# Seven products instead of eight blocks of matmuls for six of twelve pairs of the second MoE's first matrix

## The chip, the cores and the metric

The kernel runs on one core of a Trainium2 chip. The metric is the device time of one execution in microseconds (us). Before the change it is 970.91, the median of three runs (968.33 to 972.44).

## The reference, cut to what matters

Attention with decay gives x, 3072 tokens of 512 features. A gated MoE layer (512 to 1536 to 512) follows, and then the layer with which this case deals:

```python
def _moe2_ref(x, w_in, w_out, g_ln):      # x: 3072 x 512, w_in: 512 x 1024, w_out: 1024 x 512
    h = x @ w_in
    e = np.exp(h - np.max(h, axis=-1, keepdims=True))
    solu = h * (e / (np.sum(e, axis=-1, keepdims=True) + 1e-09))
    mu = np.mean(solu, axis=-1, keepdims=True)
    var = np.mean((solu - mu) ** 2, axis=-1, keepdims=True)
    ln = (solu - mu) / np.sqrt(var + 1e-06) * g_ln
    return (ln @ w_out).astype(np.float32)
```

## The kernel before

All matrices are float32, and each factor is split into a high part (fp32r, made by ScalarE) and a low part (the rest, made by VectorE); a product is three matmuls: high x high, high x low, low x high. The first stage (attention and the gate and value matrices) and the second (the MoE's down matrix) compute 2 x 2 blocks of matrices by seven products of sums (Strassen's method as Winograd ordered it) in place of eight. The second stage writes its result to `x_dram`, by GpSimd's queue (`store_x2`), while ScalarE and VectorE convert operands into a ring of seven units, ahead of TensorE.

The last stage starts at 700 us. It works on 24 blocks of 128 tokens, named (tile, block): six tiles of four. For a block there is an **up** (`both_up`: two halves of 512 features, four contractions, three matmuls each, 24 matmuls of 128x512, into a PSUM bank each) and a **down** (`both_down2`, 24 matmuls of 128x512). Between them: ScalarE copies h out of PSUM (`copy_h`, L1284), VectorE takes the row maximum (L1724), ScalarE the exponent with its sum (L1288), VectorE the softmax product (L1738) and the mean, ScalarE the sum of squares (`square_solu`, L1317) and for two blocks together the square root (`deviation_of_pair`, with an activation table load before it and before the next exponent), VectorE normalises (L1760) and transposes within 32x32 blocks into z (L1770). When all four blocks of a tile are in z, sixteen DMAs on the sync engine's queue (`move_turned`, L690) move z into `ln_t`, four for each block to come. Then ScalarE makes `ln_t_hi` (L1298), VectorE `ln_t_lo` (L1775), and TensorE does the down; ScalarE copies the result (`scale_out`, L1343) into one of two buffers, from which SP stores it (L647). Tile 0 differs: TensorE transposes its blocks by itself (L1029).

The order is written out by hand for every engine. Ups run six blocks ahead of downs. Tile 0's step does the ups of the blocks up to (2,1). From tile 1 on, step (t,j) does the up of the block `run_up_of(t, j)`, six further on, and the down of (t,j); the other engines have per step one list each in `stage_c`. The last ups, of (5,2) and (5,3), stand in the steps (4,0) and (4,1); from (4,2) on only downs are left (`tail` on ScalarE). SP's queue holds, for each tile: two loads of `x_raw` (`load_pair`, 256 tokens each), the stores of finished blocks, and the sixteen moves of the next tile; for tile 5 the moves are in two halves around the store of (4,2). z has two buffers (`z_of`), one for even and one for odd tiles; `x_raw`, `x_hi` and `x_lo` have two buffers each.

## Time and profile before

| | |
|---|---|
| median of three runs | 970.91 us |
| profiled execution | 976.88 us, its span 975.1 |
| PE busy in the span | 944.7 us (97%), 5334 matmuls |
| VectorE, ScalarE, GpSimd busy | 644.2, 521.7, 136.4 us |
| mean granted TensorE clock | 0.989 of full speed |
| last stage | from 700 to 975 us |

PE is TensorE's matmuls, PEld its weight loads, DVE VectorE, ACT ScalarE, POOL GpSimd, SP the sync engine; SPq stands for what SP's queue issues. A timeline gives the start in us from the span's start, the duration, and in brackets how long the engine was idle and for whom. Matmuls overlap in the records: their spacing is their cost.

### The profile page before, as it was taken

What the parts mean: (1) busy time and instruction counts of PE and PEld (TensorE: products, weight loads), DVE (VectorE), ACT (ScalarE), POOL (GpSimd) and SP (SyncE); (2) the same over time, 40 slices, a digit from 0 to 9 for tenths busy, and PEclk for the clock granted to TensorE, in tenths of its full rate; (3) what the DMA queues carried; (4) which work ended last, traced back from release to release, by engine and by line L of the source; (5) the groups of instructions that cost most, each with busy time, mean ns of one, the idle gap of its engine ahead of it and who ended that gap; (6) DMA issues with size and microseconds to landing.
All of it is one profiled execution on the core that took longest, in us unless ns stands there. A gap on an engine that the chain in (4) does not pass through costs nothing.

```text
span 975.1 us, 14652 instructions
## 1 busy us (share of the span) xinstructions
PE 944.7 (97%) x5334; PEld 834.8 (86%) x5334; DVE 644.2 (66%) x1065; ACT 521.7 (54%) x911; POOL 136.4 (14%) x170
## 2 busy tenths in 40 slices
PE   8979999999999999999999999999999999999996
PEld 4666787787899999999999999999888888888875
DVE  3677895786778754454679877777375766666651
ACT  3554644554556433342546554555477866666641
POOL 4313301101115430000053101010100000000000
PEclk9799999999999999999999999999999999999998
DMA  9656545626153423131364616340510054351533
GB/s 271 194 168 201 171 165 164 194 114 189 48 215 115 157 80 121 50 127 52 131 226 146 235 57 232 111 166 25 179 57 32 20 143 91 94 128 46 110 85 86
DMA packets 103847, 126.61 MB, mean 130 GB/s; under 512 B 8160, under 2 KB 84320, under 8 KB 103776
## 3 DMA queue, kind: packets, MB, share of 16 engines
q1 hardware_dynamic: 98320, 109.28, 36.5%
q0 software_dynamic: 4736, 15.73, 4.7%
q8 instruction: 43, 0.70, 0.3%
q10 hardware_dynamic: 720, 0.66, 0.2%
q14 instruction: 28, 0.23, 0.1%
HBM read 77.41 MB, written 37.75 MB: 118 GB/s over the span
## 4 chain that ended last, share of the span: by engine, by line
PE 81%; DVE 7%; DMA 3%; issue 3%; ACT 2%; SPq 2%; POOL 0%; DVEq 0%; ACTq 0%; POOLq 0%
PE psum L949 11%; PE psum L952 11%; PE psum L951 11%; PE psum L385 7%; PE psum L386 7%; PE psum L387 7%; PE psum L985 6%; PE psum L987 6%; PE psum L988 6%; PE psum L842 3%; PE psum L876 3%; PE psum L866 2%; PE psum L855 2%; SPq L690 1%; DMA out<-out_buf 1%
## 5 line engine op out<-in xcount | busy, mean ns | idle before, releaser
L949 PE MATMUL psum<-xo_hi,w_hi 128*128 128x384 f32 x560 | 194.8, 348 | 6.5 <-DVE psum L1658 2.5
L951 PE MATMUL psum<-xo_lo,w_hi 128*128 128x384 f32 x560 | 187.9, 336 | 0.0
L952 PE MATMUL psum<-xo_hi,w_lo 128*128 128x384 f32 x560 | 187.9, 336 | 0.0
L949 PEld LDWEIGHTS psum<-xo_hi,w_hi 128*128 128x128 f32 x560 | 105.7, 189 | 12.7 <-DVE c L1662 4.4
L951 PEld LDWEIGHTS psum<-xo_lo,w_hi 128*128 128x128 f32 x560 | 105.7, 189 | 0.8 <-issue 0.3
L952 PEld LDWEIGHTS psum<-xo_hi,w_lo 128*128 128x128 f32 x560 | 105.4, 188 | 0.0
L1163 ACT ACTIVATE xo_hi<-b 128x768 fp32r<-128x768 f32 x84 | 70.7, 846 | 63.2 <-PE psum L988 52.4
L1538 DVE TENSOR_TENSOR xo_lo<-b,xo_hi 128x768 fp32r<-128x768 f32 x84 | 81.3, 970 | 34.6 <-ACT xo_hi L1163 34.4
L385 PE MATMUL psum<-w_in_hi,x_hi 128*128 128x512 f32 x192 | 75.9, 395 | 2.0 <-ACT h_buf L1284 2.0
L1658 DVE TENSOR_TENSOR psum<-psum,p_buf 128x384 f32<-128x384 f32 x48 | 27.1, 565 | 76.0 <-PE psum L952 76.0
L385 PE MATMUL psum<-w_out_hi,ln_t_hi 128*128 128x512 f32 x192 | 75.1, 391 | 1.2 <-DVE ln_t_lo L1775 1.2
L386 PE MATMUL psum<-w_in_lo,x_hi 128*128 128x512 f32 x192 | 75.5, 393 | 0.0
L387 PE MATMUL psum<-w_in_hi,x_lo 128*128 128x512 f32 x192 | 75.3, 392 | 0.0
L985 PE MATMUL psum<-xo_hi,w_hi 128*128 128x384 f32 x224 | 74.8, 334 | 0.0
L987 PE MATMUL psum<-xo_lo,w_hi 128*128 128x384 f32 x224 | 74.8, 334 | 0.0
L988 PE MATMUL psum<-xo_hi,w_lo 128*128 128x384 f32 x224 | 74.8, 334 | 0.0
L386 PE MATMUL psum<-w_out_lo,ln_t_hi 128*128 128x512 f32 x192 | 74.8, 389 | 0.0
L387 PE MATMUL psum<-w_out_hi,ln_t_lo 128*128 128x512 f32 x192 | 74.7, 389 | 0.0
L1484 DVE TENSOR_TENSOR probs<-psum,mask_t 128x256 f32<-128x256 f32 x96 | 40.5, 423 | 45.4 <-PE psum L842 44.3
L1123 ACT ACTIVATE x_tile<-psum 128x128 f32<-128x128 f32 x96 | 26.4, 275 | 76.7 <-PE psum L876 65.5
L842 PE MATMUL psum<-kq_buf 128*128 128x256 f32 x192 | 60.9, 400 | 0.8 <-DMA kq_buf<-q_t 0.7
L1190 ACT ACTIVATE silu<-psum 128x384 f32<-128x384 f32 x48 | 23.5, 491 | 65.1 <-PE psum L952 64.5
(142 smaller groups left out, 2030.2 us busy)
## 6 DMA issues: line engine op xcount, KB each, us to landing
act_dram<-act_buf SPq DMA_DIRECT2D x48, 384.0 KB, 2.4
b<-act_dram SPq DMA_DIRECT2D x48, 384.0 KB, 4.8
ln_t<-z SPq DMA_DIRECT2D x80, 128.0 KB, 3.1
kq_buf<-k_t SPq DMA_DIRECT2D x32, 192.0 KB, 2.7
kq_buf<-q_t SPq DMA_DIRECT2D x64, 96.0 KB, 3.0
q_dec<-q_t SPq DMA_DIRECT2D x32, 192.0 KB, 2.5
w_raw<-weights POOLq DMA_DIRECT2D x12, 512.0 KB, 5.1
x_dram<-x_tile SPq DMA_DIRECT2D x4, 1536.0 KB, 6.0
```

Source lines behind the costliest of these rows:

```text
L385: pe.matmul(dst, w_hi, m_hi, start=start, stop=False)
L386: pe.matmul(dst, w_hi, m_lo, start=False, stop=False)
L387: return pe.matmul(dst, w_lo, m_hi, start=False, stop=stop)
L842: pe.matmul(psum[:, SCORES[ch % 2], 0:2 * P], kq_buf[:, s, i, 0:P], kq_buf[:, s, i, P:3 * P], start=True, stop=True).then_inc(scores_done, 1)
L949: pe.matmul(dst, hi[:, cols], xo_hi[:, i, kc, :], start=i in (P1, P7) and kc == 0, stop=False, skip_group_check=True)
L951: pe.matmul(dst, hi[:, cols], xo_lo[:, i, kc, :], start=False, stop=False, skip_group_check=True)
L952: mm = pe.matmul(dst, lo[:, cols], xo_hi[:, i, kc, :], start=False, stop=kc == HK - 1, skip_group_check=True)
L985: pe.matmul(dst, hi[:, cols], xo_hi[:, u, c % 2, :], start=i in (P1, P7) and c == 0, stop=False, skip_group_check=True)
L987: pe.matmul(dst, hi[:, cols], xo_lo[:, u, c % 2, :], start=False, stop=False, skip_group_check=True)
L988: mm = pe.matmul(dst, lo[:, cols], xo_hi[:, u, c % 2, :], start=False, stop=c == FC // 2 - 1, skip_group_check=True)
L1163: act.activation(xo_hi[:, u % PRODUCTS, :, :], operand(u), ACT.Copy).then_inc(d_hi_ready, 1)
L1538: dve.tensor_tensor(xo_lo[:, u % PRODUCTS, :, :], operand(u), xo_hi[:, u % PRODUCTS, :, :].bitcast(F32), ALU.subtract).then_inc(d_lo_ready, 1)
```

## The change

Blocks 12 to 23 (tiles 3, 4 and 5), six pairs, get their up by seven products of a pair: the 256 tokens and 512 contractions are a 2 x 2 of blocks on the one side, contractions and the 1024 output features on the other. A product is two contractions of three matmuls of 128x512. The pair k takes P1, P7, P6, P2, P5 in an even step and P3, P4 in the odd step behind it, in the steps where its two ups stood. The last pair (k = 5) runs all seven in its first step, (4,0), in the order P1, P7, P6, P2, P5, P4, P3, and the lists of ScalarE and VectorE for (4,0) and (4,1) are written anew.

The sums of the weights (T) are made once by GpSimd in the second stage (eight pieces of 128x512, each stored to DRAM, later loaded again and converted by ScalarE and VectorE, two at a time, in tile 0 and the steps (1,0) and (1,1)). The sums of x (S) are made by GpSimd for each pair (`make_s`, four adds of 256 columns), its conversions are 512 + 256 + 1024 columns in three parts (`s_high`, `s_low`) in place of one of 1024. Between products ScalarE copies P1 within PSUM (`copy_xy`) and P7 out of it (`copy_p7`), VectorE adds twice (`add_u3`, `add_c22`); the four quarters of h reach `h_buf` by three copies and the second sum. There is one raw buffer for x in these pairs, loaded (`load_up`) when the whole operand of the pair before is converted, and only one z: the first transposition of a tile waits until all moves of the tile before have landed. The buffers of z1, the second x2 set and `d_squares` give the room. Sums, loads and conversions not shown below follow the same form.

```diff
+        UP_ORDER = (P1, P7, P6, P2, P5, P3, P4)
+        FIRST_PAIR = 6
+        PAIRS = C_TILES * BLOCKS // 2 - FIRST_PAIR
+        S_OF = {P1: 0, P2: 1, P4: 2, P5: 3, P6: 4, P7: 5, P3: 6}
+        T_PIECES = [(p, a) for p in (P7, P6, P5, P4) for a in range(HK)]
...
+        def pair_up(t, j):
+
+            k = (t * BLOCKS + j - BLOCKS) // 2 + 5 - FIRST_PAIR
+            return k if 0 <= k < PAIRS else None
...
+        def up_done(k, i):
+            order = UP_ORDER if k < PAIRS - 1 else UP_ORDER[0:5] + (P4, P3)
+            return PRODUCTS * k + order.index(i) + 1
...
                         sp.wait_ge(x2_stored[s], DMA * 2)
+                    sp.wait_ge(t_summed, len(T_PIECES))
...
-            def load_pair(t):
-
-                for g in range(2):
-                    sp.wait_ge(x2_lo_ready, 2 * (t - 1) + g + 1)
-                    load_x2(g, t)
+            def load_up(k):
+
+                if k > 0:
+                    sp.wait_ge(s_lo_ready, 3 * k)
+                else:
+                    sp.wait_ge(x2_lo_ready, 5)
+                load_x2(0, 2, k)

             def stage_c(t):
                 if t == 0:
...
-                if t + 2 < C_TILES:
-                    load_pair(t + 2)
-                store_out(t - 1, 3)
                 for j in range(3):
+                    if j % 2 == 0 and pair_up(t, j) is not None and pair_up(t, j) + 1 < PAIRS:
+                        load_up(pair_up(t, j) + 1)
+                    if j == 0:
+                        store_out(t - 1, 3)
                     if (t, j) == (C_TILES - 2, 2):
                         move_turned(t + 1, (0, 1))
...
+                pool.tensor_tensor(t_sum[:], first, second, ALU.subtract).then_inc(t_summed, 1)
+                pool.wait_ge(t_summed, at + 1)
+                pool.dma_start(t_store(T_PIECES.index((p, a))), t_sum[:]).then_inc(t_stored, DMA)
+
+            T_SUMS = [(p, a) for a in range(HK) for p in (P5, P6, P4, P7)]
+
...
+            def make_s(k):
+
+                raw = x2_raw[0]
...
+                if k > 0:
+                    pool.wait_ge(s_lo_ready, 3 * k)
+                    pool.wait_ge(s_made, 4 * k)
+                pool.tensor_tensor(s1, a21, a22, ALU.add).then_inc(s_made, 1)
+                pool.wait_ge(s_made, 4 * k + 1)
+                pool.tensor_tensor(s2, s1, a11, ALU.subtract).then_inc(s_made, 1)
...
+            for i in range(4):
+                load_t(i)
+            make_s(0)
+            for i in range(4, len(T_PIECES)):
+                load_t(i)
+            for k in range(1, PAIRS):
+                make_s(k)


...
+            def up_product(k, i):
+
+                if i in (P1, P2):
+                    pe.wait_ge(s_lo_ready, 3 * k + 1)
+                else:
+                    pe.wait_ge(s_lo_ready, 3 * k + 3)
+                if k == 0 and i in (P4, P5, P6, P7):
+                    pe.wait_ge(t_lo_ready, T_PIECES.index((i, HK - 1)) + 1)
+                if i == P1:
+                    at_least(pe, up_c11_copied, k)
+                elif i == P7:
+                    at_least(pe, up_c21_copied, k)
+                elif i in (P6, P2):
+                    pe.wait_ge(up_xy_copied, k + 1)
+                elif i in (P5, P4):
+                    pe.wait_ge(up_u3_ready, k + 1)
+                else:
+                    pe.wait_ge(up_c22_ready, k + 1)
+                dst = psum[:, {P1: UX, P2: UX, P7: UV, P4: UV}.get(i, UY), :]
+                for a in range(HK):
+                    x_hi, x_lo = s_hi[:, S_OF[i] * HK + a, :], s_lo[:, S_OF[i] * HK + a, :]
+                    m_hi, m_lo = up_weight(i, a)
+                    pe.matmul(dst, x_hi, m_hi, start=i in (P1, P7) and a == 0, stop=False, skip_group_check=True)
+                    pe.matmul(dst, x_hi, m_lo, start=False, stop=False, skip_group_check=True)
+                    mm = pe.matmul(dst, x_lo, m_hi, start=False, stop=a == HK - 1, skip_group_check=True)
+                mm.then_inc(up_product_done, 1)
+
...
-                        both_up(*run_up_of(t, j))
+                    if (t, j) in ((1, 0), (1, 1)):
+                        both_up(2, j + 2)
+                    if pair_up(t, j) is not None:
+                        whole = pair_up(t, j) == PAIRS - 1
+                        for i in (UP_ORDER[0:5], UP_ORDER[5:7])[j % 2] if not whole else (UP_ORDER[0:5] + (P4, P3), ())[j % 2]:
+                            up_product(pair_up(t, j), i)
                     both_down2(t, j)
...
+            def s_high(k, part):
+
+                raw = x2_raw[0]
+                if k == 0:
+                    act.wait_ge(h_done, 4 * FIRST_PAIR)
+                else:
+                    act.wait_ge(up_product_done, up_done(k - 1, P2 if part == 0 else P4))
+                if part < 2:
...
                         tail(t, j)
                         continue
-                    if j > 0:
+                    if pair_up(t, j) is None:
+                        if j > 0:
+                            scale_out(t, j - 1)
+                        both_high(t, j)
+                        square_solu(2, j + 1)
+                        if j == 0:
+                            deviation_of_pair(2, 0)
+                        if j == 0:
+                            for i in (4, 5):
+                                t_high(i)
+                        copy_h(2, j + 2, 0)
+                        copy_h(2, j + 2, 1)
+                        if j == 1:
+                            for part in range(3):
+                                s_high(0, part)
+                        exponent(2, j + 2)
+                        if j == 1:
+                            for i in (6, 7):
+                                t_high(i)
+                        continue
+                    k = pair_up(t, j)
+                    a, b = blocks_of(k)
+                    if j % 2 == 0:
+                        if j > 0:
+                            scale_out(t, j - 1)
+                        elif t > 1:
+                            scale_out(t - 1, 3)
+                        copy_xy(k)
+                        both_high(t, j)
+                        copy_p7(k)
+                        square_solu(*last_of(k))
+                        deviation_of_pair(last_of(k)[0], last_of(k)[1] // 2)
+                        copy_up(k, P2, UX, 0, 0, up_c11_copied)
+                        if k + 1 < PAIRS:
+                            s_high(k + 1, 0)
+                        else:
+                            copy_up(k, P4, UV, 1, 0, up_c21_copied)
+                            copy_up(k, P3, UY, 0, 1, up_c12_copied)
+                            both_high(t, j + 1)
+                            exponent(*a)
+                        continue
+                    if k + 1 == PAIRS:
+                        exponent(*b)
+                        square_solu(*a)
                         scale_out(t, j - 1)
-                    elif t > 1:
-                        scale_out(t - 1, 3)
+                        both_high(*next_block(t, j))
+                        continue
                     both_high(t, j)
-                    last_up = (t + 1, j + 1) if j < 3 else (t + 2, 0)
-                    square_solu(*last_up)
-                    if j % 2 == 0:
-                        deviation_of_pair(t + 1, j // 2)
-                    copy_h(*run_up_of(t, j), 0)
-                    if run_up_of(t, j) == LAST_BLOCK:
-                        both_high(*next_block(t, j))
-                    if j % 2 == 1 and t + 2 < C_TILES:
-                        x2_high(t + 2, j // 2)
-                    copy_h(*run_up_of(t, j), 1)
-                    exponent(*run_up_of(t, j))
+                    scale_out(t, j - 1)
+                    copy_up(k, P3, UY, 0, 1, up_c12_copied)
+                    copy_up(k, P4, UV, 1, 0, up_c21_copied)
+                    exponent(*a)
+                    s_high(k + 1, 1)
+                    s_high(k + 1, 2)
+                    exponent(*b)
+                    square_solu(*a)

             def tail(t, j):

...
                     for i in range(PARTS):
-                        at_least(dve, ln_t_moved[i], DMA * PARTS * (t - 2))
-                dve.transpose(z_of(t)[:, :, :, j, :].rearrange("p k f c -> p (k f) c"),
+                        at_least(dve, ln_t_moved[i], DMA * PARTS * (t - 1))
+                dve.transpose(z[:, :, :, j, :].rearrange("p k f c -> p (k f) c"),
...
                             both_low(*next_block(t, j))
                         continue
+                    if pair_up(t, j) is None:
+                        both_low(t, j)
+                        if j == 0:
+                            invert_pair(2, 0)
+                        turn_up(2, j)
+                        if j == 0:
+                            for i in (4, 5):
+                                t_low(i)
+                        row_max(2, j + 2)
+                        if j == 1:
+                            for part in range(3):
+                                s_low(0, part)
+                        take_up(2, j + 2)
+                        if j == 1:
+                            for i in (6, 7):
+                                t_low(i)
+                        continue
+                    k = pair_up(t, j)
+                    a, b = blocks_of(k)
+                    if k + 1 == PAIRS and j % 2:
+                        both_low(t, j)
+                        row_max_up(k, 1)
+                        take_up(*a)
+                        both_low(*next_block(t, j))
+                        take_up(*b)
+                        continue
                     both_low(t, j)
+                    if j % 2 == 0 and k + 1 == PAIRS:
+                        add_u3(k)
+                        add_c22(k)
+                        invert_pair(last_of(k)[0], last_of(k)[1] // 2)
+                        turn_up(last_of(k)[0], last_of(k)[1] - 1)
+                        row_max_up(k, 0)
+                        turn_up(*last_of(k))
+                        continue
                     if j % 2 == 0:
-                        invert_pair(t + 1, j // 2)
-                    turn_up(t + 1, j)
-                    row_max(*run_up_of(t, j))
-                    if run_up_of(t, j) == LAST_BLOCK:
-                        both_low(*next_block(t, j))
-                    if j % 2 == 1 and t + 2 < C_TILES:
-                        x2_low(t + 2, j // 2)
-                    take_up(*run_up_of(t, j))
+                        add_u3(k)
+                        invert_pair(last_of(k)[0], last_of(k)[1] // 2)
+                        add_c22(k)
+                        turn_up(last_of(k)[0], last_of(k)[1] - 1)
+                        turn_up(*last_of(k))
+                        s_low(k + 1, 0)
+                        continue
+                    row_max_up(k, 0)
+                    row_max_up(k, 1)
+                    take_up(*a)
+                    s_low(k + 1, 1)
+                    s_low(k + 1, 2)
+                    take_up(*b)

             tiles(stage_c)
```

## Rows read from the trace of the kernel before

**Rows 1.** Busy time by windows, tiles 1 to 4 of the last stage (columns in the first line).
```profile
core 0: us, PE busy (x) PEld busy (x) DVE busy (x) ACT busy (x) POOL busy (x), PEclk, DMA share, GB/s
820.00:840.00 20.00, 20.00 (x90) 16.57 (x89) 13.63 (x22) 13.47 (x21) 0.00 (x0) 1.00 0.72 174
```

**Rows 2.** Timeline of PE, first matmuls of the steps (2,3) and (4,0): start, duration, instruction.
```profile
857.17 0.39 PE L385 MATMUL psum<-w_in_hi,x_hi 128*128 128x512 f32 x1
...
911.57 0.39 PE L385 MATMUL psum<-w_in_hi,x_hi 128*128 128x512 f32 x1
```

**Rows 3.** Timelines of PE, DVE and SP around the down of block (1,0).
```profile
785.60 0.39 PE L387 MATMUL psum<-w_in_hi,x_lo 128*128 128x512 f32 x1
786.27 0.50 PE L385 MATMUL psum<-w_out_hi,ln_t_hi 128*128 128x512 f32 x1 [0.28 <-DVE ln_t_lo L1775]
...
785.54 1.28 DVE L1775 TENSOR_TENSOR ln_t_lo<-ln_t,ln_t_hi 128x512 fp32r<-128x512 f32 x2
...
777.40 12.22 SPq L690 DMA_DIRECT2D ln_t<-z  x16
```

**Rows 4.** Timelines of DVE, SP, PE and ACT at the end.
```profile
936.25 1.25 DVE L1770 STREAM_TRANSPOSE z<-solu 128x1024 f32<-128x1024 f32 x1
...
937.52 6.95 SPq L690 DMA_DIRECT2D ln_t<-z  x8
...
953.36 15.62 SPq L647 DMA_DIRECT2D out<-out_buf  x5
...
945.27 0.50 PE L385 MATMUL psum<-w_out_hi,ln_t_hi 128*128 128x512 f32 x1 [0.91 <-DVE ln_t_lo L1775]
...
967.82 0.60 ACT L1343 ACTIVATE out_buf<-psum 128x512 f32<-128x512 f32 x1 [3.57 <-DMA out<-out_buf]
```

**Rows 5.** Groups by line and form: busy us, mean ns, idle before and releaser.
```profile
L1284 ACT ACTIVATE h_buf<-psum 128x512 f32<-128x512 f32 x48 | 28.1, 590 | 19.2 <-PE psum L387 19.0
L1298 ACT ACTIVATE ln_t_hi<-ln_t 128x512 fp32r<-128x512 f32 x40 | 23.3, 624 | 12.8 <-DMA ln_t<-z 12.8
L1277 ACT ACTIVATE x_hi<-x_raw 128x1024 fp32r<-128x1024 f32 x12 | 12.6, 1048 | 0.0
L1288 ACT ACTIVATE e_buf<-h_buf,neg_max 128x1024 f32<-128x1024 f32 x24 | 27.7, 1153 | 18.5 <-DVE neg_max L1724 18.4
L1775 DVE TENSOR_TENSOR ln_t_lo<-ln_t,ln_t_hi 128x512 fp32r<-128x512 f32 x40 | 26.1, 687 | 34.3 <-ACT ln_t_hi L1298 34.3
L1720 DVE TENSOR_TENSOR x_lo<-x_raw,x_hi 128x1024 fp32r<-128x1024 f32 x12 | 14.6, 1217 | 0.0
L1770 DVE STREAM_TRANSPOSE z<-solu 128x1024 f32<-128x1024 f32 x20 | 24.9, 1245 | 0.7
L1724 DVE TENSOR_REDUCE neg_max<-h_buf 128x1 f32<-128x1024 f32 x24 | 29.0, 1206 | 21.1 <-ACT h_buf L1284 21.0
L1738 DVE SCALAR_TENSOR_TENSOR solu<-h_buf,e_inv,e_buf 128x1024 f32<-128x1024 f32 x24 | 30.8, 1285 | 0.9
```

**Rows 6.** Timelines of POOL and DVE in the second stage.
```profile
509.98 0.73 POOL L761 TENSOR_TENSOR w_raw<-w_raw 128x256 f32<-128x256 f32 x1 [2.57 <-DMA w_raw<-weights]
...
511.06 1.49 DVE L1523 TENSOR_TENSOR b<-b 128x768 f32<-128x768 f32 x1
...
590.25 0.54 POOL L820 DMA_DIRECT2D x_dram<-act_buf  x1 [23.38 <-ACT act_buf L1225]
```

**Rows 7.** The tile ln_t, its moves from 777 to 790.
```profile
DMA to landing us min/median/max: 2.6/3.0/3.9
```

**Rows 8.** Timeline of PE behind the gap at the start of the last stage.
```profile
707.06 0.67 PE L385 MATMUL psum<-w_in_hi,x_hi 128*128 128x512 f32 x1 [1.82 <-ACT h_buf L1284]
```

**Rows 9.** Busy time by windows at the same place (columns as in rows 1).
```profile
708.00:709.00 1.00, 1.00 (x4) 0.81 (x3) 1.00 (x2) 0.47 (x1) 0.00 (x0) 0.50 0.04 16
```

**Rows 10.** The tile x_raw, its loads at 829 to 831 and at 696 to 698.
```profile
DMA to landing us min/median/max: 5.6/5.9/6.3
...
DMA to landing us min/median/max: 9.8/10.3/10.7
```

**Rows 11.** Group by line and form, second stage, 532 to 700.
```profile
L1523 DVE TENSOR_TENSOR b<-b 128x768 f32<-128x768 f32 x9 | 8.6, 952 | 0.3 <-DMA b<-act_dram 0.3
```

189 lines of the change are left out of this document (173 added, 16 removed).

## The prediction

> **What bounds the kernel now.** I read the page first (TensorE, PE, is busy for nearly the whole span), then busy time by windows in the last stage, where the change lies, then the timelines around its two gaps. In seven windows of 20 us from 800 to 940, of which one stands here, PE is never idle, at a granted clock of 1.00, while VectorE (DVE) and ScalarE (ACT) have a third of their time free [rows 1]. There a step (one block up, one block down, 48 matmuls) lasts (911.57 - 857.17) / 5 = 10.88 us, so a 128x512 matmul costs 0.2267 us [rows 2]. The last stage is bound by PE except in two places. The first is the down of block (1,0): its ups end at 785.83 and it starts at 786.27, 0.44 us late, for the conversion that VectorE begins at 785.54 [rows 3]. The second is the end. The last block transposition of tile 5 ends at 937.50; then come eight moves by DMA, one store, eight moves, and only then the stores that wait behind them on the same queue. PE waits 0.91 us for the first four moves, ScalarE waits 3.57 us for a store before its last copy at 967.82, and the last store lands at the span's end, 975.1 [rows 4]. So the end follows that transposition by 37.6 us. PE's own last matmul ends at 945.27 + 4 x 5.44 + 0.2 = 967.2, 0.6 us before that copy, and it hangs on the moves as well.
>
> **Part 1, matmuls removed.** A pair of blocks takes 7 x 2 x 3 = 42 matmuls of the same shape for its up instead of 48. Six pairs save 36, or 36 x 0.2267 = 8.2 us of PE. Five pairs (6.8 us) come before the step (4,0) in which the last pair runs; the sixth lies inside it.
>
> **Part 2, work added beside.** Per pair ScalarE gets one more copy from PSUM (0.59) and conversions of 1792 columns instead of 1024. From the rows of 512 and 1024 columns (0.62 and 1.05) and an estimate of 0.37 for 256, that is +1.0 us. VectorE gets two sums (0.70 each, estimated from the 512-column row of 0.69) and 1.1 us more of low parts, +2.5 us [rows 5]. Over a pair of 20.4 us both stay near 80% busy. What counts is the order, so I walked one pair through the queues, from the start of its even step. PE: P1 0, P7 1.36, P6 2.72, P2 4.08, P5 5.44, down 6.80; odd step P3 12.24, P4 13.60, down 14.96, next pair 20.40. ScalarE's odd step ends with table load, exponent a, two conversions, exponent b, square a, then a store copy. Its copy of P1 is ready 2.3 us into the next pair, 0.4 ahead of P6. VectorE's last low part of the next operand is ready 1.2 us in, 0.2 ahead of P7; the sum U3 is ready at 5.0, 0.4 ahead of P5; the odd step's ln_t_lo 2 us ahead. So I cost the steady pairs at **nothing**, but the margins are thin: without them each 0.1 us costs 0.5 us over five pairs.
>
> **Part 3, GpSimd (POOL) in the second stage.** Eight sums of 512 columns cost about 1.46 each (an estimate, twice the 0.73 of a 256-column add), 0.54 to issue [rows 6], and 3.0 to 3.9 to land, as the moves do [rows 7]: 5 to 6 us each. The first four fit into the 23.38 us in which GpSimd waits for ScalarE [rows 6]; the other four delay stores by some 6 us. ScalarE reuses those slots 5 to 10 us later and the operand ring is seven units ahead, so they cost PE nothing. Were the ring's cover gone, it would be the 2 to 3 us by which one slot comes free late.
>
> **Part 4, conversions of the T pieces, and one z.** In tile 0 the two T conversions before exponent(2,0) put 1.04 us on ScalarE and 1.22 on VectorE into the chain that ends in the down of (1,0). Waits of 0.5 to 0.6 us in that chain absorb most, and the gap there grows by **0.3 us**. Then the single z. The transposition of (2,0) now waits until all sixteen moves of tile 1 have landed. They are issued from 777.40 to 789.62 [rows 3] and land 3.0 us after issue [rows 7], so at 792.1; before it ran at 789.6 into the other z. Behind it stand transposition 1.25, two T pieces 1.22, row maximum 1.20, exponent 1.24, softmax and mean 1.85 and the first ln_t_lo 0.69, with semaphores 799.5 [rows 5]. PE would reach the down of (1,1) at 786.27 + 0.3 + 5.44 + 5.44 = 797.45. That is a new gap of **2.1 us**. In later tiles the moves are done before the transposition's turn: its turn comes 7.7 us into an even step of 12.2, the last move lands at about 7.7 too, within 0.4. The clock stays at its upper level (2.4 GHz) in this sum: behind the gap of 0.91 us at 945.27 [rows 4] the matmuls kept their spacing.
>
> **Part 5, the last pair.** Step (4,0) starts 6.8 - 0.3 - 2.1 = 4.4 us earlier. From its start, before: second half's copy, row maximum, exponent, softmax, then norm and transposition, the last ends 25.9 in (937.50 - 911.57). After: P3 ends at 9.7, its copy at 10.3, row maximum a 11.6, the waiting transposition of (5,1) 13.6, ln_t_lo of (4,1) 14.9, row maximum b 16.0, take_up a 17.7. Then VectorE waits for ln_t_hi of (4,2), which on ScalarE stands behind exponent b, square a and a store: 20.5. Two ln_t_lo 21.3, take_up b 23.0, and two norms with transpositions end at 27.4. So the chain is **1.5 us longer**, though both blocks' products were done 6 us sooner. PE finds gaps before the downs of (4,2) and (4,3), 0.3 and 2 us, but they cost nothing: down (5,0) waits for the moves anyhow.
>
> **Sum:** 6.8 - 0.3 - 2.1 - 1.5 = 2.9 us earlier at the last transposition, and the end follows by the same 37.6 us. The sixth pair's matmuls and the gaps at (4,2), (4,3) vanish in that wait. The profiled execution took 976.88 and should take 974.0; it stands 6.0 above the median of the runs shown, so on the median of 970.91 this makes **968.0 us**. A measurement of this kernel can tell some 0.5%, 4.9 us, from no change.
>
> **Rival 1, the clock.** After PE's gap of 1.82 us before 707.06 the granted clock fell to 0.50 (1.2 GHz): eight matmuls at 0.43 us, 8 x 0.20 = 1.6 us [rows 8, 9]. The new gap of 2.1 us is as long, and those at (4,3) and (5,0) come near it. Against it: ahead of 797 PE runs over 10 us without a gap. If it falls there, the gain is 1.3 us: 969.6.
>
> **Rival 2, the gain is kept.** If the moves land sooner or the end is less tied to the queue when nobody profiles, PE's saving shows in full, up to 8.2 us: 962.7; half way, 965.5. For it: the chain before the transposition has waits for single releasers that may shorten, and 6 us between profiled and median time are unexplained. Against it: the end in the trace hangs on the moves, and the last chain is longer.
>
> **Rival 3, slower: the load of the next pair.** With one raw buffer, ScalarE converts the next pair's x ahead of ln_t_hi of the odd block, and the load is issued behind sixteen moves, 4 us into the even step. ln_t_hi is needed by 14.2. A landing time over 8.5 us stalls PE by the excess, in tiles 2 and 3, and the delay returns with the next moves. Loads in that place took 5.6 to 6.3 us, the pair at 696.7 took 9.8 to 10.7 [rows 10]. At 10.7 the walk gives stalls of 4 us at each of (2,1) and (3,1) and 1.6 of small ones, 9.6 in all: 2.9 - 9.6 = 6.7 slower, 977.6. It decides from 9.2 us on, and passes 0.5% at 10.3.
>
> **Rival 4, GpSimd's sums in each pair.** Four adds of 256 columns, 0.73 alone. With them beside it, VectorE's 768-column subtraction took 1.49 [rows 6] against 0.95 alone [rows 11]. In my walk they run 7 to 13 us into the even step, where VectorE has 2 us before PE needs it: four times 0.54 is 2.2, nothing to speak of. If each add holds VectorE for its whole 0.73 instead, that is 2.9 us a pair, 0.9 over the slack, 4.6 over five pairs: 972.6. This is the rule of the Trainium skill (SBUF — State Buffer, Who interferes with whom): a VectorE instruction with two SBUF inputs contends with a GpSimd one that reads SBUF, and the later one blocks fully; the 0.54 of this trace is less, and may be an add met half way.
>
> **Chances.** Forecast 0.47 (of it 0.06 faster than 0.5% by scatter alone); rival 1 0.21; rival 2 0.17, all faster; rival 3 0.09, slower; rival 4 0.06, a third of it slower with other margins gone. So faster 0.23, slower 0.11, within 0.5% 0.66. The range reaches from rival 2's upper end, 963, past rivals 1 and 4 to 974.5; left out are rival 3 and the top of rival 2. The forecast's own range is 965.5 to 970.5, by landing times of 2.6 to 3.9 us [rows 7] and the thin margins.
>
> **What would show it.** Right: pairs 20.4 us apart from (1,2) to (4,0); VectorE idle before the transposition of (2,0) on a ln_t move; a PE gap of about 2 us before the down of (1,1), clock 1.00 behind it; last transposition 27.4 us after step (4,0) starts and 37.6 before the end; PE gaps at (4,2) and (4,3). Wrong: PE waits inside the products (P7, P6 or P5), ScalarE waiting for x_raw beyond 14 us into an even step, or an end that doesn't follow the last transposition.

## The result, and where the forecast went

Five runs of the changed kernel gave 972.13 to 976.15 us, median **975.48**, against 970.38 for five of the kernel before; the ratio on record is 1.0033, with a 95% interval of 1.0017 to 1.0050. It was measured twice more, twelve runs each: 1.0032 (1.0013 to 1.0050) and 1.0026 (1.0012 to 1.0041). The ratio is not the quotient of the two medians, which lie 5.1, 3.7 and 2.1 us apart in the three groups; I go by the ratios and their intervals. By them the change costs 2.5 to 3.2 us where 2.9 us of gain were forecast (968.0, with a range of 963 to 974.5), though 36 of TensorE's matmuls, some 8.2 us of its work, are gone as planned (5298 in the profile instead of 5334).

The profiled execution took 972.98 us, its span is 971.2. It can't be held against the first profile of the kernel before: that one held 1.82 us idle and eight slow matmuls at 707 [rows 8, 9], and a second profile of the same kernel (below) has 0.86 us there and no slow ones. The early part of the span differs as well, though neither kernel's code differs there. The last stage's first matmul starts at 695.4 to 696.5 in the three profiles of the kernel before and its variant (run 2), and at 691.4 to 695.2 in the fifteen profiles of the changed kernel and its variants. Most of this is there by the first matmul with `xo_hi`, at 51.4 to 53.8 against 49.3 to 51.2. That is no mere scatter, as all three stand above all fifteen. Its cause was not tested, and no run shows whether executions without a profile have it too. So I compare the **last stage alone**, from its first matmul to the span's end, and what this gives can't be added up to the whole time: 278.7 us in the first profile of before, **275.4** in the second; 278.1, 277.9 and 276.5 in the three of the changed kernel.

Busy time by windows in the changed kernel, the columns as in [rows 1]; this row answers to it:

```profile
820.00:840.00 20.00, 20.00 (x88) 16.17 (x87) 16.29 (x26) 14.36 (x26) 3.62 (x4) 1.00 0.61 145
```

PE is full here, as forecast. VectorE went from 13.6 to 16.3 us of 20, and GpSimd's sums are new. Its timeline around the downs of (1,0) and (1,1), which answers to [rows 3]:

```profile
780.77 0.50 PE L466 MATMUL psum<-w_out_hi,ln_t_hi 128*128 128x512 f32 x1 [1.49 <-DVE ln_t_lo L2046]
...
794.85 0.50 PE L466 MATMUL psum<-w_out_hi,ln_t_hi 128*128 128x512 f32 x1 [2.88 <-DVE ln_t_lo L2046]
...
796.36 0.62 PE L466 MATMUL psum<-w_out_hi,ln_t_hi 128*128 128x512 f32 x1
796.77 0.63 PE L467 MATMUL psum<-w_out_lo,ln_t_hi 128*128 128x512 f32 x1
797.20 0.63 PE L468 MATMUL psum<-w_out_hi,ln_t_lo 128*128 128x512 f32 x1
...
879.62 0.50 PE L466 MATMUL psum<-w_out_hi,ln_t_hi 128*128 128x512 f32 x1 [0.74 <-DVE ln_t_lo L2046]
```

The new gap before (1,1) stands where it was forecast. The engine was idle for 2.88 us, and the down starts 3.1 us later behind that of (1,0) than before. From 796.36 on, 1.5 us behind the gap, the matmuls go 0.43 us apart, eight of them: 1.6 us more. The granted clock of 795 to 805 is 0.83 (1.2 GHz for a third of it, else 2.4 GHz). What leads to the gap, on VectorE, ScalarE and SP:

```profile
783.24 0.81 DVE L2031 TENSOR_SCALAR solu<-solu,mean,rstd 128x1024 f32<-128x1024 f32 x1
787.47 1.25 DVE L2041 STREAM_TRANSPOSE z<-solu 128x1024 f32<-128x1024 f32 x1 [3.41 <-DMA ln_t<-z]
788.63 1.25 DVE L2063 TENSOR_TENSOR t_lo<-t_stage,t_hi 128x512 fp32r<-128x512 f32 x2
789.80 1.21 DVE L1995 TENSOR_REDUCE neg_max<-h_buf 128x1 f32<-128x1024 f32 x1
...
794.11 1.28 DVE L2046 TENSOR_TENSOR ln_t_lo<-ln_t,ln_t_hi 128x512 fp32r<-128x512 f32 x2
...
791.05 1.15 ACT L1472 ACTIVATE e_buf<-h_buf,neg_max 128x1024 f32<-128x1024 f32 x1 [4.73 <-DVE neg_max L1995]
...
771.39 11.57 SPq L773 DMA_DIRECT2D ln_t<-z  x16
...
774.83 1.14 POOL L956 DMA_DIRECT2D t_stage<-act_dram  x2 [18.00 <-DVE t_lo L2063]
```

The transposition of (2,0) waits 3.41 us for the one z. Behind it in VectorE's list stand two low parts of T and the maximum, behind that ScalarE's exponent waits 4.73 us, and behind both stands the ln_t_lo for which PE waits. From the transposition's start to PE's down it is 7.4 us, as the forecast had it. What it had wrong is the landing. The tile ln_t, its moves from 770 to 783, answers to [rows 7] (3.0 in the middle, 3.9 at most), and under it the same view of the last two of them alone:

```profile
DMA to landing us min/median/max: 2.6/5.2/6.2
...
DMA to landing us min/median/max: 5.1/5.1/5.1
```

Two loads of T pieces, 256 KB each, are issued by GpSimd at 774.83, between these moves. Now the last pair and the end, on PE, DVE, SP and ACT, answering to [rows 2, 4]:

```profile
905.60 0.39 PE L1196 MATMUL psum<-w_in_hi,s_hi 128*128 128x512 f32 x1
...
927.00 0.50 PE L466 MATMUL psum<-w_out_hi,ln_t_hi 128*128 128x512 f32 x1 [0.71 <-DVE ln_t_lo L2046]
...
934.33 0.50 PE L466 MATMUL psum<-w_out_hi,ln_t_hi 128*128 128x512 f32 x1 [1.60 <-DVE ln_t_lo L2046]
...
932.46 1.25 DVE L2041 STREAM_TRANSPOSE z<-solu 128x1024 f32<-128x1024 f32 x1
...
933.73 6.85 SPq L773 DMA_DIRECT2D ln_t<-z  x8
...
949.58 15.90 SPq L728 DMA_DIRECT2D out<-out_buf  x5
...
964.31 0.60 ACT L1570 ACTIVATE out_buf<-psum 128x512 f32<-128x512 f32 x1 [3.59 <-DMA out<-out_buf]
```

The last transposition ends at 933.71, 28.1 us after the pair's first product (25.9 before, 27.4 forecast), and the end follows it by 37.5 us. The account by stretches of the last stage, in us (the columns "forecast" and "measured" give differences to the kernel before):

| stretch | before, second profile | changed, three profiles | forecast | measured |
|---|---|---|---|---|
| first matmul to down (1,0) | 87.40 | 87.69, 86.95, 88.00 | +0.3 | -0.5 to +0.6 |
| to down (1,1) | 11.01 | 14.08, 14.52, 14.02 | +2.1 | +3.0 to +3.5 |
| to first up matmul of (4,0) | 114.24 | 110.75, 110.61, 109.10 | -6.8 | -3.5, -3.6, -5.1 |
| to end of last transposition | 25.92 | 28.11, 28.32, 27.63 | +1.5 | +1.7 to +2.4 |
| to the span's end | 36.9 | 37.5, 37.5, 37.8 | 0 | +0.6 to +0.9 |
| sum | 275.4 | 278.1, 277.9, 276.5 | -2.9 | +2.7, +2.5, +1.1 |

The profiled executions of the changed kernel (972.98, 973.04 and 972.08) are 1.5 to 2.5 us faster than the medians of their groups, so they show rather too little of the loss.

### The profile page after: what moved, and what is told of

It reads as the page before. It is cut to its first block, busy times and chain, and to the rows that moved or that the text cites. A ratio compares the mean times of both kernels' runs of the same rounds, so it can differ in the third digit from the quotient of the medians.

```text
span 971.2 us, 14811 instructions
## 1 busy us (share of the span) xinstructions
PE 935.9 (96%) x5298; PEld 825.3 (85%) x5298; DVE 671.0 (69%) x1097; ACT 532.1 (55%) x937; POOL 180.0 (19%) x219
## 4 chain that ended last, share of the span: by engine, by line
PE 61%; DVE 12%; DMA 7%; SPq 7%; issue 5%; ACT 5%; POOL 2%; DVEq 0%; ACTq 0%; POOLq 0%
PE psum L1102 10%; PE psum L1105 10%; PE psum L1104 10%; SPq L773 6%; PE psum L1140 6%; PE psum L1138 6%; PE psum L1141 6%; PE psum L995 3%; PE psum L1029 2%; PE psum L1019 2%; DMA x_raw<-x_dram 2%; DMA ln_t<-z 2%; PE psum L1008 2%; DVE z L2041 1%; PE psum L466 1%
## 5 line engine op out<-in xcount | busy, mean ns | idle before, releaser
L1809 DVE TENSOR_TENSOR xo_lo<-b,xo_hi 128x768 fp32r<-128x768 f32 x84 | 84.2, 1006 | 28.0 <-ACT xo_hi L1347 27.5
L862 POOL TENSOR_TENSOR q_dec<-q_dec,q_decay_t 128x384 f32<-128x384 f32 x32 | 33.9, 1061 | 167.2 <-DMA q_dec<-q_t 120.7
L1374 ACT ACTIVATE silu<-psum 128x384 f32<-128x384 f32 x48 | 23.6, 491 | 65.3 <-PE psum L1105 64.7
L1370 ACT ACTIVATE silu<-psum 128x384 f32<-128x384 f32 x48 | 23.6, 492 | 56.0 <-PE psum L1105 55.6
L466 PEld LDWEIGHTS psum<-w_out_hi,ln_t_hi 128*128 128x128 f32 x192 | 36.3, 189 | 19.8 <-DVE ln_t_lo L2046 11.6
```

The costliest lines, as they stand in the source:

```text
L466: pe.matmul(dst, w_hi, m_hi, start=start, stop=False)
L1809: dve.tensor_tensor(xo_lo[:, u % PRODUCTS, :, :], operand(u), xo_hi[:, u % PRODUCTS, :, :].bitcast(F32), ALU.subtract).then_inc(d_lo_ready, 1)
```

## The experiments

Medians differ a little between groups of runs, so each is given beside that of the kernel before in its own group (23 to 29 runs each).

**1. The kernel before, profiled again.** No edit.

> The kernel before, profiled once more. Its first profile ran 976.9 us, above all of its other runs (968.3 to 972.4), and holds an idle 1.98 us of the PE at 707 us with eight slow matmuls behind it (1.6 us), which the profile of the changed kernel lacks. Theory 1 (that stretch is chance, worth about 3.5 us): this profile shows less than 1 us idle there, no slow matmuls, and ends some 3.5 us sooner, at about 971. Theory 2 (it belongs to the kernel before, and the change removes it): the same 1.98 and 1.6 us are there again.

Span 971.9 (973.65 us in all), and PE at the start of the last stage, at (1,0) and at (5,0):

```profile
705.71 0.50 PE L385 MATMUL psum<-w_in_hi,x_hi 128*128 128x512 f32 x1 [0.86 <-ACT h_buf L1284]
...
783.87 0.50 PE L385 MATMUL psum<-w_out_hi,ln_t_hi 128*128 128x512 f32 x1 [0.28 <-DVE ln_t_lo L1775]
...
942.69 0.50 PE L385 MATMUL psum<-w_out_hi,ln_t_hi 128*128 128x512 f32 x1 [0.77 <-DVE ln_t_lo L1775]
```

Theory 1: what the first profile's last stage had more, 3.3 us, was not there again, and the total fell by 3.2. The forecast was made as a difference, so this doesn't account for its error, but it is why the first profile can't serve for the comparison.

**2. One z alone**, in the kernel before:

```diff
-            return z1 if t % 2 else z0
+            return z1
...
-                        at_least(dve, ln_t_moved[i], DMA * PARTS * (t - 2))
+                        at_least(dve, ln_t_moved[i], DMA * PARTS * (t - 1))
```

> The kernel before with one part of the change alone: one buffer z for the turned blocks instead of two, so that the first transposition of each later tile waits for the moves of the tile ahead. Theory 1 (the shared z is the larger part of what ate the gain): a new idle time of the PE of 2 to 3 us at the down projection of block (1,1), and 2 to 4.5 us more in all, according to whether the clock falls behind it. Theory 2 (without the pieces of T, their loads and sums, the moves land in 3 us instead of 5 to 6, and the wait is short): idle under 1 us there, total within 1 us of before.

971.74 beside 971.77, ratio 1.0000 (0.9990 to 1.0011). The moves landed in 3.1 us, and the wait is there, yet short:

```profile
787.78 1.25 DVE L1770 STREAM_TRANSPOSE z<-solu 128x1024 f32<-128x1024 f32 x1 [1.95 <-DMA ln_t<-z]
```

From down (1,0) to (1,1) it took 11.41 us instead of 11.01. The single z alone costs nothing that reaches the end: theory 2.

**3. The transposition of (2,0) later**, with its norm, behind the maximum of (2,2), in the changed kernel:

```diff
-                        turn_up(2, j)
+                        if j == 1:
+                            turn_up(2, j)
                         if j == 0:
                             for i in (4, 5):
                                 t_low(i)
                         row_max(2, j + 2)
+                        if j == 0:
+                            turn_up(2, j)
```

> The changed kernel with the transposition of block (2,0) put behind the maximum of block (2,2) in VectorE's order, so that the wait for z holds up neither that maximum nor the exponent that follows it on ScalarE. Theory 1 (the wait for z costs because of the work behind it): the idle 3.0 us at the down projection of (1,1) falls to 1 us or less, the eight slow matmuls behind it go, and the total falls by 3.5 to 4.5 us, to about 971. Theory 2 (something else is late there, such as the landing of the moves or the sums on ScalarE): the idle time stays above 2 us, total within 1 us.

968.73 beside 971.77, ratio 0.9967 (0.9954 to 0.9979): this one change of order turns the loss into a gain. VectorE now waits behind the maximum:

```profile
783.07 1.22 DVE L1995 TENSOR_REDUCE neg_max<-h_buf 128x1 f32<-128x1024 f32 x1 [0.19 <-ACT h_buf L1468]
784.21 0.80 DVE L2031 TENSOR_SCALAR solu<-solu,mean,rstd 128x1024 f32<-128x1024 f32 x1
787.74 1.25 DVE L2041 STREAM_TRANSPOSE z<-solu 128x1024 f32<-128x1024 f32 x1 [2.73 <-DMA ln_t<-z]
788.90 0.11 DVE L2002 TENSOR_SCALAR e_sum_eps<-e_sum 128x1 f32<-128x1 f32 x1
```

The wait for z ends no sooner (four T loads were issued from 772.85 to 783.7 here, and the moves took 5.6 us in the middle), but the exponent has run meanwhile and the softmax starts 1.2 us behind the transposition's start instead of 4.9. The gap at (1,1) was 1.41 us, the clock stayed at 1.00. Theory 1, with a larger fall of the total than it expected, and a gap somewhat over the 1 us that it expected.

**4. The last pair split like the others** (five products in (4,0), two in (4,1), the same lists as the five pairs ahead), in the changed kernel:

```diff
-            order = UP_ORDER if k < PAIRS - 1 else UP_ORDER[0:5] + (P4, P3)
+            order = UP_ORDER
...
-                        for i in (UP_ORDER[0:5], UP_ORDER[5:7])[j % 2] if not whole else (UP_ORDER[0:5] + (P4, P3), ())[j % 2]:
+                        for i in (UP_ORDER[0:5], UP_ORDER[5:7])[j % 2]:
```

> The changed kernel with the last pair run as the five pairs ahead of it: five products in the first step and two in the second, and the other engines' order the same as theirs. Theory 1 (the end follows the last transposition, and what sets that is the chain behind the last pair's products): the last transposition comes later by the work that moves behind the down projection of (4,0), about 3 us, some 3 us slower in all. Theory 2 (the new order of the last pair lengthened the chain and ate part of the gain): 1 to 2 us faster. Theory 3 (neither matters): within 0.5 us.

974.46 beside 971.77, ratio 1.0022 (1.0010 to 1.0035); the changed kernel stood at 1.0026 to 1.0033. The chain to the last transposition is 28.8 us instead of 28.1. The intervals of the two overlap. None of the three theories at full size, theory 3 nearest: running all seven products at once, with the lists as they were written, gained nothing that can be told.

**5. The changed kernel again.** No edit.

> The changed kernel once more, beside the others of this group. Theory 1 (its profile is typical of the third stage): from the first matmul of the third stage to the end 278 us as in its first profile, against 275.4 in the second profile of the kernel before, with idle times of 1.5 and 3 us at the down projections of (1,0) and (1,1) and eight slow matmuls; total 3 us above the kernel before. Theory 2 (the falls of the clock behind (1,1) are chance): no slow matmuls this time, 276.5 us.

974.51 beside 970.83, ratio 1.0032. Idle 0.96 at (1,0) and 3.32 at (1,1), eight slow matmuls, last stage 277.9: theory 1.

**6. Without the T pieces in the last stage** (what takes their place in the products are pieces of the weight):

```diff
-            for i in range(4):
-                load_t(i)
             make_s(0)
-            for i in range(4, len(T_PIECES)):
-                load_t(i)
...
-                    for i in (0, 1):
-                        t_high(i)
...
-                    for i in (0, 1):
-                        t_low(i)
```

> The changed kernel with its one z and its list of transpositions, but without the eight pieces of T in the third stage: neither loaded nor converted, and four of the seven products take pieces of the weight in their place (same matmuls, other values in the output). Theory 1 (the pieces, beside the moves in the queues and ahead of the maxima on VectorE and ScalarE, are what makes the wait for z and the idle times long): idle at (1,0) back to under 0.5 us and at (1,1) under 1 us, no slow matmuls, total 5 to 6 us below the changed kernel, near 970. Theory 2 (the one z alone does it): idle at (1,1) still 2 us or more, total at most 2 us lower.

968.66, 2.2 below the kernel before of its group (ratio 0.9976, 0.9963 to 0.9989) and **5.9 below the changed kernel** (5.4 by the ratios); last stage 272.9, idle time at (1,0) 0.28 us as in the kernel before. PE at (1,1):

```profile
791.62 0.50 PE L464 MATMUL psum<-w_out_hi,ln_t_hi 128*128 128x512 f32 x1 [0.65 <-DVE ln_t_lo L2032]
```

Theory 1.

**7. The same, with two z** in the place of four pieces:

```diff
-            t2_hi = sb(c, "t2_hi", [P, HK, BANK], F32R)
+            z0 = sb(c, "z0", [P, F2C, PARTS, BLOCKS, 32])
...
-                        at_least(dve, ln_t_moved[i], DMA * PARTS * (t - 1))
+                        at_least(dve, ln_t_moved[i], DMA * PARTS * (t - 2))
```

> As the run without the pieces of T, and with two buffers z again (in the place of four of the pieces). Theory 1 (the one z costs little once the pieces are gone): within 1 us of the run without the pieces. Theory 2 (the one z costs by itself, at (1,1) and at the last pair, where the transposition of (5,0) waited 1.5 us for it): 2 to 3 us below that run.

965.97, 2.7 below run 6 (1.9 by the ratios, 0.9956 with 0.9941 to 0.9971, whose interval overlaps that of run 6 a little). Last stage 270.6 instead of 272.9, no idle time at (1,1) and (3,1) and 0.22 us at (4,2), the chain of the last pair 27.6. Theory 2, at its lower end: with seven products one z does cost, some 2 us, spread over (1,1), the wait at (3,1) and the last pair. In the kernel before (run 2) it cost nothing.

**8. The lists of the last pair written anew**, on top of edit 3; VectorE's even and odd step, and ScalarE's odd step:

```diff
-                        turn_up(last_of(k)[0], last_of(k)[1] - 1)
+                        normalize(last_of(k)[0], last_of(k)[1] - 1)
+                        row_max_up(k, 1)
+                        turn_blocks(last_of(k)[0], last_of(k)[1] - 1)
                         row_max_up(k, 0)
+                        both_low(t, j + 1)
                         turn_up(*last_of(k))
...
-                        both_low(t, j)
-                        row_max_up(k, 1)
                         take_up(*a)
-                        both_low(*next_block(t, j))
                         take_up(*b)
+                        both_low(*next_block(t, j))
...
                         exponent(*b)
-                        square_solu(*a)
                         scale_out(t, j - 1)
                         both_high(*next_block(t, j))
+                        square_solu(*a)
```

(ScalarE's first exponent waits for both maxima, as they now come in the other order.)

> The changed kernel with the later transposition of (2,0), and with the lists of the last pair written once more: the maximum of (5,3) ahead of the transposition that waits for z, the two exponents back to back, both of VectorE's sums of the last pair ahead of the low part of (4,2), and ScalarE's scaling of (4,0) and high part of (4,2) in front of its squares. Theory 1 (the end follows the last transposition by 37.6 us, and the chain of the last pair to it is 28.2 us, 2.3 longer than before): the chain falls to 25 us, and the total by 3 us against the run with the later transposition alone, to about 965.5. Theory 2 (the end is set by the matrix engine or by the stores): the chain shortens and the total stays within 1 us of that run.

965.99 beside 970.83, ratio 0.9953 (0.9935 to 0.9971, five runs). The chain is 24.90 us instead of 28.1, and the end follows by 37.4, as theory 1 has it. The total is only 1.4 to 1.9 us below edit 3 alone (0.9967 here, 0.9973 in run 14), where 3 were expected, and the intervals overlap: by itself this run doesn't settle it. Run 13 does, below.

**9. All conversions of T, but only two of the eight loads** (the other six pieces are converted from what these two left):

```diff
-            for i in range(4):
+            for i in range(2):
                 load_t(i)
             make_s(0)
-            for i in range(4, len(T_PIECES)):
-                load_t(i)
...
-                act.wait_ge(t_loaded[i % 2], DMA * (i // 2 + 1))
+                act.wait_ge(t_loaded[i % 2], DMA)
```

> The changed kernel with all sixteen conversions of the pieces of T, but only the first two of their eight loads (the other six pieces are made from what those two left, so their values differ). Without any piece the third stage lasted 272.9 us instead of 278. Theory 1 (the loads cost: they stand beside the moves in the queues, so that the moves land in 5 to 6 us instead of 3 to 4): the wait of the transposition of (2,0) ends some 2 us sooner, idle at (1,1) 1 us or less, no slow matmuls, total 3.5 to 4.5 us below the changed kernel. Theory 2 (the conversions cost, 2.4 us on ScalarE and VectorE for each two pieces, ahead of the maximum and the exponent): idle at (1,1) still 2.5 to 3 us, total within 1 us.

970.26 beside 970.31, ratio 0.9997 (0.9986 to 1.0009), so **2.8 to 3.5 us better than the changed kernel** (1.0026 to 1.0033, in other groups). Last stage 274.1. The moves and the gap:

```profile
DMA to landing us min/median/max: 2.6/3.0/3.9
```

```profile
791.88 0.50 PE L466 MATMUL psum<-w_out_hi,ln_t_hi 128*128 128x512 f32 x1 [1.31 <-DVE ln_t_lo L2044]
```

Theory 1, at a little less than its size: six loads more or fewer, nothing else, decide whether the moves take 3.0 or 5.2 us. The last move lands 3.9 us after its issue starts, instead of 5.1, and the clock stays at 1.00. Of the 5.4 to 5.9 us of run 6 some 3 are the loads; that leaves 2 to 3 for the conversions (a difference between groups, not a run of its own).

**10. Without GpSimd's work in the second stage.**

```diff
-                if t == 1:
+                if t == B:
                     for at in range(first, last):
...
-            load_b22()
```

> The changed kernel without what it added to the second stage: no load of b22, none of GpSimd's eight differences there, no stores of them (the third stage loads and converts what lies in the store, so its values differ). Theory 1 (that work is hidden, as forecast): within 0.7 us of the changed kernel, and the third stage as long as its 278 us. Theory 2 (it takes VectorE's access, whose subtractions there grew from 970 to 1006 ns): 1 us or more faster.

974.03 beside 970.31, ratio 1.0040 (1.0028 to 1.0052); last stage 277.6. That is no faster than the changed kernel (1.0026 to 1.0033). Theory 1: the work was hidden, though its sums of 512 columns took 1.46 to 2.07 us where 1.46 were estimated.

**11. Without GpSimd's sums in the pairs:**

```diff
-                    rows, src = slice(KC + HK, PRODUCTS * HK), s_raw[:]
+                    rows, src = slice(KC + HK, PRODUCTS * HK), raw[:].rearrange("p k (h n) -> p (k h) n", n=P)
```

(`make_s` returns ahead of its waits and adds, and VectorE's low parts read the same block.)

> The changed kernel without GpSimd's four sums for each pair of the third stage (the operands that they make are taken from the raw block instead, so the values differ). Theory 1 (they hold VectorE up only where it has time): within 0.7 us of the changed kernel. Theory 2 (each holds VectorE for its own length, 24 of them at 0.7 to 1.1 us, a part of it ahead of down projections): the idle 0.75 us at (3,1) goes, and the end comes 1.5 us or more sooner.

971.96 beside 970.31, ratio 1.0014 (1.0005 to 1.0022). That is 1 to 2 us better than the changed kernel, but the intervals overlap, and in this one profile the clock did not fall behind 3.53 us of idle time, which by itself makes 1.6 us. At (3,1) the wait for z is there and the idle time of PE is not:

```profile
872.72 1.25 DVE L2030 STREAM_TRANSPOSE z<-solu 128x1024 f32<-128x1024 f32 x1 [1.88 <-DMA ln_t<-z]
...
877.39 0.40 PE L466 MATMUL psum<-w_out_hi,ln_t_hi 128*128 128x512 f32 x1
```

What the sums cost in all is not settled: between nothing and 2 us.

**12. Loads of the last four pieces held back** until the moves of tile 1 have landed, on top of run 8, with the conversions of pieces 4 to 7 a step later:

```diff
             make_s(0)
+            for i in range(PARTS):
+                pool.wait_ge(ln_t_moved[i], DMA * PARTS)
             for i in range(4, len(T_PIECES)):
                 load_t(i)
```

> The run with the lists of the last pair written anew (966.0 us), with the loads of the last four pieces of T held back until the moves of tile 1 have landed, and their conversions put one step later. Theory 1 (loads beside the moves are what makes them slow): the transposition of (2,0) waits 1 us or less instead of 1.8, the moves land in 4 us, idle at (1,1) none, 0.5 to 1.5 us faster. Theory 2: nothing is gained at (1,1), or the pieces are late for the products of the first pair: same or slower by 1 us.

965.61 beside 970.31, ratio 0.9949 (0.9935 to 0.9962); run 8 stood at 0.9953. The moves landed in 3.0 us and the idle time at (1,1) went, as theory 1 has it, but edit 3 had already made that wait cheap: in time it is theory 2, nothing gained that can be told.

**13 to 16. One group of four:** the new lists of run 8 alone, edit 3 alone, edits 3, 8 and 12 together, and the changed kernel.

> The changed kernel with the lists of the last pair written anew, and nothing else. Theory 1 (the end follows the last transposition, so that the chain's 28.2 us against 25.9 before reach it whole): from the last pair's first product to the end of the last transposition 24.9 us, and the total 3.3 us below the changed kernel of this group. Theory 2 (another wait takes the place of the chain's in part): the chain is 24.9 us and the total falls by less than 2 us.

> The changed kernel with the later transposition of (2,0) alone, once more, now beside the list alone. Theory 1 (idle time and slow matmuls at (1,1) reach the end whole): 3.5 to 5 us below the changed kernel of this group. Theory 2: less than 2.5 us.

> The changed kernel with all three edits: the later transposition, the lists of the last pair, the pieces' loads held back until the moves have landed. Theory 1 (the parts add up): 8 to 9 us below the changed kernel of this group and some 5 below the kernel before. Theory 2 (they overlap): 6 to 7 us below the changed kernel.

> The changed kernel, for the comparison in this group: 3 to 3.7 us above the kernel before, a third stage of 278 us, the chain of the last pair 28.2 us.

| run | median | median against the changed kernel's | ratio to before (971.6) |
|---|---|---|---|
| changed kernel | 973.65 | | 1.0026 (1.0012 to 1.0041) |
| new lists alone | 971.0 | -2.7 | 1.0000 (0.9989 to 1.0011) |
| edit 3 alone | 968.64 | -5.0 | 0.9973 (0.9960 to 0.9987) |
| all three | 966.77 | -6.9 | 0.9948 (0.9928 to 0.9968) |

With the new lists alone the chain is 24.91 us, against 27.63 in this group's profile of the changed kernel: 2.7 us less, and 2.7 less in all (2.5 by the ratios). Its two ends, the first product of the last pair and the last transposition:

```profile
906.78 0.39 PE L1196 MATMUL psum<-w_in_hi,s_hi 128*128 128x512 f32 x1
...
930.44 1.25 DVE L2041 STREAM_TRANSPOSE z<-solu 128x1024 f32<-128x1024 f32 x1
```

Theory 1. PE at the downs of (4,2) and (4,3) had no idle time left over 0.25 us. Edit 3 alone gives 5.0 us, theory 1; in this second profile of it the transposition waited 0.72 us and PE had no idle time at (1,1). Its last stage took 273.4 us against 276.5, so the profiles hold 3.1 of the 5.0. All three edits together give 6.9, not 8 to 9: theory 2 by its number, though the two parts measured here make 7.7, and with six runs of it 6.9 and 7.7 can't be told apart. In that profile one gap was back, 0.92 us at (3,1), and (1,0) had 1.44.

The clock: this is the changed kernel's third profile at (1,1), with no slow matmul behind a gap nearly as long as the first one's.

```profile
795.80 0.50 PE L466 MATMUL psum<-w_out_hi,ln_t_hi 128*128 128x512 f32 x1 [2.80 <-DVE ln_t_lo L2046]
...
797.06 0.39 PE L468 MATMUL psum<-w_out_hi,ln_t_lo 128*128 128x512 f32 x1
```

A single profile can't say how often the clock falls, but the mean granted clock of every execution is on record. For the changed kernel it is 0.9921 (29 executions; 0.9916, 0.9917 and 0.9927 by group), for the kernel before 0.9939 to 0.9947 by group, and 0.9951 and 0.9944 in the two runs of edit 3, without a long gap. In the two groups in which both kernels were measured, the changed kernel stands 0.0025 and 0.0017 below the kernel before. An estimate from this: these shares of 971 us are 2.4 and 1.7 us, so that the clock is a large part of the loss in the executions without a profile as well.

## Why the forecast was wrong, step by step

**Part 1 holds.** 36 matmuls less at 0.2267 us. In the first profile the stretch from (1,1) to (4,0) is 110.75 us instead of 114.24; with the 1.6 us of slow clock, 0.9 at (3,1) and 0.8 in pauses of at most 0.2 us taken off, it is the 6.8 that was reckoned.

**Part 4 is the step that failed.** The forecast let the moves "land 3.0 us after issue", taken from a trace in which nothing else was on the way. The change itself puts two 256 KB loads between them, and with these the moves took 5.2 us in the middle (5.4 and 4.8 in the other two profiles) and the last one 5.1 (5.6 and 4.9) from the start of its issue, against 3.9 before. That makes the down of (1,1) 3.0 to 3.5 us late instead of 2.1. Run 9 shows the cause: without the loads it is 3.0 us in the middle and 3.9 for the last again, and a gap of 1.31 us. I had counted the T pieces' conversions and not their loads. (The forecast's own sum is loose here: 789.62 is the end of the last issue, which starts at 787.8, and 3.0 behind 789.62 is 792.6, not 792.1. So its time for z held 4.3 us for the last move, and 5.1 was still more. That the gap came out within 1.4 us of the forecast owes something to this.) The Trainium skill (DMA: Bandwidth & Descriptors, Issuing engines are not separate DMA queues) says that DMAs of the scalar, sync and GpSimd engines end up on the same DMA engines and interleave. By that rule the loads had to be counted, and run 9 agrees.

The term of 0.3 us for the conversions at (1,0) was too small as well. PE sat idle there for 0.96 to 1.49 us instead of 0.28, so 0.7 to 1.2 more; without loads it was 0.78 (run 9), without T pieces 0.28 (run 6). The stretch ahead of (1,0) grew by less only because other small waits in it differ.

The same step had also named all that stands behind the waiting transposition, two T pieces, the maximum, exponent, softmax, and took it as fixed. Run 3 shows what that order cost: 5 to 6 us between two kernels whose lists differ in one place. (The loads' 3 us and the order's 5 don't add up, as both act by the same wait.) And that in later tiles the last move lands within 0.4 us of the transposition's turn was wrong in all three: the transpositions waited 1.08, 1.83 and 1.21 us in the steps (2,0), (3,0) and (4,0). VectorE and GpSimd in step (3,0):

```profile
874.00 1.25 DVE L2041 STREAM_TRANSPOSE z<-solu 128x1024 f32<-128x1024 f32 x1 [1.83 <-DMA ln_t<-z]
875.17 1.28 DVE L2031 TENSOR_SCALAR solu<-solu,mean,rstd 128x1024 f32<-128x1024 f32 x1
...
878.35 1.82 DVE L2046 TENSOR_TENSOR ln_t_lo<-ln_t,ln_t_hi 128x512 fp32r<-128x512 f32 x2
...
875.99 1.07 POOL L969 TENSOR_TENSOR s_raw<-s_raw,x_raw 128x256 f32<-128x256 f32 x1
```

**Rival 1 came true.** The clock fell to 1.2 GHz behind the gap at (1,1) in two of the changed kernel's three profiles, at the 1.6 us that it had priced, and the granted clocks of all executions say the same (1.7 to 2.4 us by the estimate above). The forecast gave it 0.21 and kept the clock at its upper level behind 2.1 us of idle time, though it had seen it fall behind 1.82; it argued from a gap of 0.91 us, behind which it stayed. The mis-sized landing made the gap longer still.

**Part 2, put at nothing, cost 1.5 us**, as much as the clock did in a profile. The pairs' first products are 20.40, 20.72, 20.45, 21.54 and 20.40 us apart, forecast 20.4. 0.9 us of it is the time lost before (3,1), the rest pauses of under 0.25 us; no product waited longer than that. At (3,1) it seems to take two things, the wait for z and GpSimd's sums beside VectorE: with two z and the sums (run 7) PE had no idle time there, and with one z, the same wait and no sums (run 11) it had none either. With both it was between nothing and 0.93 us, in one profile each. The forecast's figure for ScalarE, +1.0 us per pair, leaves out the copy's 0.59; no other step used it.

**Part 5, mis-sized.** +1.5 forecast, +1.7 to +2.4 measured. A term left out is the wait for z in the last pair, 1.21 us before the transposition of (5,0); with two z (run 7) the chain was 27.6, near the forecast. The gaps at (4,2) and (4,3), 0.3 and 2 us forecast, were 0.71 and 1.60. The statement that the end follows the last transposition holds in every profile, 36.9 to 37.8 us, whatever was done to PE, and run 13 bears it out in the total. That is why the sixth pair's matmuls bring nothing, and why 2.7 us off the chain bring 2.7 us.

**Part 3 holds** (run 10). **Rival 3**, the late x, did not come: the loads behind the moves landed in 5.0 and 4.7 us, those in the steps between in 8.0, all under the 9.2 from which it was to decide. ScalarE did wait 4.33 us for one at 875.18, but its ln_t_hi was done at 876.9, ahead of VectorE, which came to the low parts at 878.35 only. **Rival 4**: beside GpSimd's sums VectorE's norm took 1.28 us instead of 0.81 and a pair of low parts 1.82 instead of 1.29 (2.36 where two sums met it, at 836.3, 855.8 and 897.5), and GpSimd's own sum 1.07 instead of 0.74. The rule of the Trainium skill (SBUF — State Buffer, Who interferes with whom) has the later of the two wait for the whole of the other; these rows show 0.33 to 0.54 us for each sum met, less than a whole sum, and what it comes to in the total stays open (run 11).

**The sum.** Forecast -2.9. The stretch to (1,0) -0.8 to +0.3, the mis-sized landing +0.9 to +1.4, the clock +1.6 in two profiles of three, the pairs +1.6 to +1.7, the last chain +0.2 to +0.9, the end +0.6 to +0.9: together 4.0 to 5.6 in the three profiles, which makes +1.1 to +2.7 for the last stage. The term of the end is the difference to the second profile of before; against the 37.6 us that the forecast took, the end was right within 0.2. By the ratios the error is 5.4 to 6.1 us, and the landing's direct share of it is the smaller part. The larger part is what the longer gap brought with it, the clock, and the terms beside it, the pairs and the last chain.

## What to carry to other kernels

A wait that a change adds is priced at the landing time of its transfer as it will be, with the loads that the same change puts beside it, not as the old trace shows it. Where an engine has to wait on a transfer, put behind that wait only what needs it: here one norm and its transposition moved behind one maximum were worth 5 us, more than half of what 36 matmuls less could bring. Where a profile of the same kernel shows the clock fall behind a gap, a new gap as long is priced with that fall. And where the end hangs on a chain of other engines, only that chain's length counts: of the two versions with all seven products in hand early, the one whose lists used them was 2.7 us faster.

The version with all three edits runs at 0.9948 of the kernel before (0.9928 to 0.9968; another group gave 0.9949), 4.7 to 4.8 us faster than it and 6.9 faster than the changed kernel.

## What the hardware showed beyond the forecast

Behind idle times of PE of 2.6 to 3.7 us at (1,1) the clock fell in five profiles and stayed in two (3.53 us in run 11, 2.80 in the changed kernel's third). A fall cost seven or eight matmuls at 0.43 us, 1.6 us, and eleven, 2.2 us, in run 4. It also fell behind 1.82 us [rows 8] and 2.23 us (run 4, at (4,2)), and in no profile behind the gaps of 0.9 to 1.6 us.

Sixteen moves of 128 KB landed in 3.0 to 3.1 us in the middle when alone (eight profiles) and in 4.7 to 5.6 with two to four loads of 256 KB among or right behind them (ten profiles).
